# Attention, routed experts and a gated layer in one kernel: the first heads are split and loaded in another order, the row constants are cleared elsewhere, the first expert's row list is worked out inside the last attention steps, and one activation table set serves exponential and logarithm

## The reference

```python
def _attn_ref(q, k, v, tau):              # q, k, v: 4 x 8 heads x 576 x 64
    scores = scale * np.matmul(q, k.transpose(0, 1, 3, 2))
    thresh = np.max(scores, axis=-1, keepdims=True) - tau
    scores = np.where(scores >= thresh, scores, -1000000000.0)
    scores = scores - np.max(scores, axis=-1, keepdims=True)
    attn = np.exp(scores)
    attn = attn / (np.sum(attn, axis=-1, keepdims=True) + 1e-09)
    return np.matmul(attn, v)

def _moe_ref(x, w_gate, w_noise, noise, w1, w2):   # x: 2304 x 512, 8 experts of width 1024
    noise_scale = np.log1p(np.exp(x @ w_noise))
    noisy_logits = x @ w_gate + noise_scale * noise
    top2 = np.argpartition(-noisy_logits, 2, axis=1)[:, :2]
    ...
            h = np.maximum(x[mask] @ w1[e], 0.0)
            out[mask] += top2_w[mask, k, None] * (h @ w2[e])

def _moe2_ref(x, w_in, w_out, alpha):              # 2304 x 512, hidden width 2048
    h = x @ w_in
    g = np.maximum(h, 0.0) + alpha * np.minimum(h, 0.0)
    return g @ w_out
```

## Time and profile before

| what | value |
|---|---|
| runs, median | 1287.92 us (1285.68 to 1288.28, 3 runs) |
| the profiled execution's own time | 1287.75 us |
| its span, first to last instruction | 1285.5 us |
| busy: PE, PEld, DVE, ACT, POOL | 96%, 88%, 49%, 42%, 44% |
| first matmul of the kernel starts | 15.55 us after the span's start |
| last product of attention starts | 375.51 us |
| first expert matmul starts | 394.74 us |

### The profile page before, as it was taken

One profiled execution on the slowest core, in us unless ns is written; L12 is line 12 of the kernel. 1 busy time (PEld: TensorE's weight loads), 2 busy tenths in 40 slices (PEclk: granted clock), 3 DMA queues, 4 the chain that ended last, 5 costly groups with the idle time before them and its releaser, 6 DMA issues.

```text
span 1285.5 us, 20211 instructions
## 1 busy us (share of the span) xinstructions
PE 1232.2 (96%) x7666; PEld 1127.0 (88%) x7666; DVE 626.0 (49%) x1256; ACT 537.0 (42%) x957; POOL 569.6 (44%) x409
## 2 busy tenths in 40 slices
PE   4999999999988999999999999999999999999998
PEld 4899999999977789989999998998998999999997
DVE  6888888888777321121112121226455446445443
ACT  5777777777764333333333333323222112111211
POOL 5999999999651544352534434354510101000000
PEclk9999999999988999999999999999999999999999
DMA  5545454544421344342523434343221102000000
GB/s 172 133 123 138 124 142 122 139 123 122 139 68 58 102 144 132 99 138 92 164 76 119 122 123 132 113 153 121 90 67 49 33 1 74 16 0 24 17 1 24
DMA packets 71408, 123.11 MB, mean 96 GB/s; under 512 B 11936, under 2 KB 30880, under 8 KB 71328
## 3 DMA queue, kind: packets, MB, share of 16 engines
q1 hardware_dynamic: 57856, 87.69, 23.9%
q0 software_dynamic: 6080, 19.93, 4.9%
q10 hardware_dynamic: 7392, 14.42, 3.0%
HBM read 82.43 MB, written 19.92 MB: 80 GB/s over the span
## 4 chain that ended last, share of the span: by engine, by line
PE 79%; POOL 7%; ACT 4%; DMA 3%; DVE 3%; issue 3%; SPq 0%; ACTq 0%; DVEq 0%; POOLq 0%
PE h_ps L756 32%; PE y_ps L773 10%; PE y_ps L774 10%; PE y_ps L775 10%; PE o_acc L614 4%; POOL probs_lo L1429 4%; PE ring L565 2%; DMA qk_parts<-qk_parts 2%; PE t_ps L734 2%; PE ring L566 2%; PE ring L579 2%; PE ring L578 2%; POOL qk_parts L1434 1%; ACT probs_hi L867 1%; ACT qk_parts L875 1%
## 5 line engine op out<-in xcount | busy, mean ns | idle before, releaser
L756 PE MATMUL h_ps<-x_hi,region_a 128*128 128x384 f32 (+1 forms) x1408 | 340.0, 314 | 4.3 <-DVE x_lo L1325 4.3
L756 PEld LDWEIGHTS h_ps<-x_hi,region_a 128*128 128x128 f32 x1408 | 245.0, 189 | 10.1 <-DVE x_lo L1325 5.0
L1429 POOL TENSOR_TENSOR probs_lo<-probs,probs_hi 128x576 fp32r<-128x576 f32 x160 | 227.1, 1428 | 45.4 <-ACT probs_hi L867 45.2
L756 PE MATMUL h_ps<-x_lo,region_a 128*128 128x384 f32 (+1 forms) x704 | 219.3, 311 | 0.0
L1335 DVE SCALAR_TENSOR_TENSOR h_lo<-h_ps,h_hi 128x256 fp32r<-128x256 f32 (+1 forms) x128 | 62.7, 491 | 305.5 <-ACT h_hi L970 305.5
L973 ACT ACTIVATE h_hi<-act_out 128x384 fp32r<-128x384 f32 (+1 forms) x112 | 53.7, 480 | 305.9 <-DVE act_out L1346 305.9
L773 PE MATMUL y_ps<-region_b,h_hi 128*128 128x512 f32 x436 | 172.5, 396 | 1.4 <-DVE h_lo L1352 1.4
L775 PE MATMUL y_ps<-region_b,h_lo 128*128 128x512 f32 x436 | 170.8, 392 | 0.0
L774 PE MATMUL y_ps<-region_b,h_hi 128*128 128x512 f32 x436 | 170.7, 392 | 0.0
L1415 POOL TENSOR_TENSOR region_b<-stage,region_b 128x1024 fp32r<-128x1024 f32 x40 | 95.9, 2399 | 140.6 <-ACT region_b L848 140.5
L970 ACT ACTIVATE h_hi<-h_ps 128x256 fp32r<-128x256 f32 (+1 forms) x128 | 55.9, 437 | 237.7 <-PE h_ps L756 233.3
(11 more groups left out here) (247 smaller groups left out, 2404.4 us busy)
## 6 DMA issues: line engine op xcount, KB each, us to landing
stage<-in_moe_w SPq DMA_DIRECT2D x56, 512.0 KB, 3.7
qk_parts<-qk_parts SPq DMA_DIRECT2D x120, 160.0 KB, 2.5
qk_raw<-in_qk SPq DMA_DIRECT2D x32, 320.0 KB, 3.3
expert_rows<-rows_out ACTq DMA_DIRECT2D x8, 768.0 KB, 3.6
v_nat<-in_v SPq DMA_DIRECT2D x16, 320.0 KB, 3.2
early<-in_moe_w SPq DMA_DIRECT2D x16, 256.0 KB, 4.8
...
```

Source lines behind the costliest of these rows:

```text
L756: mm = pe.matmul(h_ps[:, c % 2, 0:width], wt, x[kind][:, cc, :], start=(n == 0), stop=(n == 3 * C - 1))
L1429: pool.tensor_tensor(probs_lo[:, m % 4, :], probs[:, m % 4, :], probs_hi[:, m % 4, :].bitcast(F32), ALU.subtract).then_inc(lo_done, 1)
```

## The change

1. **Filling.** Heads 0, 1 and 2 are split at slots -14, -13 and -11. The clearing of the constant rows of heads 2 and 3 goes from DVE to POOL, under a semaphore of its own (`later_row_consts`) for which PE waits only from head 2 on. The wait for `tau` goes from DVE's beginning to slot -4, and no longer counts in `consts_v`. ACT's last copy of a head moves one slot behind its split. SP loads the second pair of heads right after the first; the second pair's values and the fourth eighth of the weights come later. The weight eighths are split at other slots.
2. **Draining.** Pairs of row tiles are turned one slot earlier (`PAIR_AT` 144 in place of 145), while the first pairs are loaded in the same slot as before, 138. POOL writes its constants in slots 152 and 154. The counts (slot 162) go through a free place of `ring` and stand ahead of the turning of the last head. DVE works out the places in slots 161 to 163. Only two of the late turns stand ahead of the sum now, the rest behind it, and they wait for `first_idx_ready`.
3. **Table set.** ACT loads the set with exponential and logarithm once, at its beginning.

The diff, cut to its core:

```diff
-    PAIR_AT = TILES - 3 * NT
+    PAIR_AT = TILES - 16
...
-        SPLIT_AT = {-14: ((0, 0), (0, 1)), -9: ((1, 0), (1, 1)), -3: ((2, 0), (2, 1)), 2: ((3, 0),), 3: ((3, 1),)}
+        SPLIT_AT = {-10: ((0, 0), (0, 1)), -8: ((1, 0), (1, 1)), -1: ((2, 0),), 1: ((2, 1),), 3: ((3, 0),), 4: ((3, 1),)}
+        LOAD_FIRST_AT = {-5: 3}
+        FIRST_SPLITS = {-14: 0, -13: 1, -11: 2}
+        FIRST_COPIES = {-10: 2}
...
+        FIRST_COUNTS_AT = TILES - 1 + LAG
+        last_use = use("om", 0, NH + 1)
+        first_ps, marks_ps = (ring[:, (last_use + 1) % 3, a, :] for a in range(2))
...
             load_pair(0, 0)
+            load_pair(0, 2)
+            load_first_weights(0)
             sp.dma_start(threshold[:, :], tau.partition_broadcast(P)).then_inc(tau_in, 16)
-            load_first_weights(0)
             load_v_pair(0, 0)
-            load_pair(0, 2)
             load_first_weights(1)
             load_first_weights(2)
-            load_v_pair(0, 2)
-            load_first_weights(3)
...
-                for n, pairs in ((PAIR_AT - 7, range(0, 2)), (PAIR_AT - 1, range(2, PAIRS))):
+                for n, pairs in ((PAIR_AT - 6, range(0, 2)), (PAIR_AT - 1, range(2, PAIRS))):
...
             pe.wait_ge(consts, 2)
-            pe.wait_ge(consts_v, 3)
+            pe.wait_ge(consts_v, 2)
             pe.wait_ge(max_row_consts, 2)
...
                         wait(pe, copies_in[s % 2], copied(head(i, g)))
+                        pe.wait_ge(later_row_consts, 2)
...
+                if tile(i, c) == FIRST_COUNTS_AT:
+                    pe.wait_ge(freed, last_use - 1)
+                    pe.wait_ge(route_pool, 2)
+                    pe.wait_ge(first_mask_ready, 1)
+                    pe.matmul(first_ps[:, 0:FIRST_TILES], lower[:, :], first_mask[:, :], start=True, stop=False)
...
             pe.wait_ge(x_in[0], 16)
-            for k in range(4):
-                turn_late(k)
+            turn_late(0)
+            turn_late(1)
             pe.wait_ge(first_tokens_ready, 2)
...
             mm.then_inc(first_summed, 1)
+            pe.wait_ge(freed, past("om", 0, NH + 1))
+            pe.wait_ge(first_idx_ready, 1)
+            turn_late(2)
+            turn_late(3)
...
-                    if head(i, g) < BY_ENGINES:
-                        act.wait_ge(qk_hi_done, head(i, g) + 1)
-                        act.activation(k_ones[0:D, g % U, :], q_hi2[D:P, g % U, :].bitcast(F32), ACT.Copy).then_inc(highs_moved, 1)
-                        act.wait_ge(lows_moved, head(i, g) + 1)
-                        act.wait_ge(highs_moved, head(i, g) * 2 + 1)
-                        act.activation(k_parts[0:D, g % U, :], k_ones[0:D, g % U, :].bitcast(F32), ACT.Copy).then_inc(highs_moved, 1)
+                last = FIRST_SPLITS.get(tile(i, c) - 1)
+                if last is not None and last < BY_ENGINES:
+                    act.wait_ge(lows_moved, last + 1)
+                    act.wait_ge(highs_moved, last * 2 + 1)
+                    act.activation(k_parts[0:D, last, :], k_ones[0:D, last, :].bitcast(F32), ACT.Copy).then_inc(highs_moved, 1)
+                if g is not None and 0 <= head(i, g) < BY_ENGINES:
+                    act.wait_ge(qk_hi_done, head(i, g) + 1)
+                    act.activation(k_ones[0:D, g % U, :], q_hi2[D:P, g % U, :].bitcast(F32), ACT.Copy).then_inc(highs_moved, 1)
...
+            act.preload_act_table_set("natural_log_exp_and_others")
...
-            dve.wait_ge(tau_in, 16)
-
-            dve.tensor_scalar(threshold[:, :], threshold[:, :], -1.0 / SCALE, None, ALU.mult).then_inc(consts_v, 1)
...
+                if tile(i, c) == -4:
+                    dve.wait_ge(tau_in, 16)
+                    dve.tensor_scalar(threshold[:, :], threshold[:, :], -1.0 / SCALE, None, ALU.mult).then_inc(threshold_ready, 1)
...
                     if head(i, g) == BY_ENGINES - 1:
-                        max_rows_cleared(slice(2, U))
                         dve.wait_ge(max_row_consts, 2)
...
-                if tile(i, c) == FIRST_LOGITS_AT + 3:
+                if tile(i, c) == FIRST_COUNTS_AT - 1:
                     first_choice()
+                if tile(i, c) == FIRST_COUNTS_AT:
+                    first_expert_slots()
+                if tile(i, c) == FIRST_COUNTS_AT + 1:
+                    first_expert_places()
...
+            pool.memset(q_lo[D:D + 4, 2:U, :].bitcast(F32), 0.0).then_inc(later_row_consts, 1)
+            pool.memset(k_ones[D:D + 4, 2:U, :].bitcast(F32), 1.0).then_inc(later_row_consts, 1)
...
+                if tile(i, c) == PAIR_AT + 8:
+                    pool.wait_ge(pair_turned, 2)
+                    pool.memset(ones_bf[:, :], 1.0).then_inc(route_pool, 1)
```

180 lines of the change are left out of this document (94 added, 86 removed).

## The result

The changed kernel takes **1277.77 us** (median of 4 runs, 1276.27 to 1278.40) against 1287.80 us for the kernel before on the same chip (1285.68 to 1288.28): a ratio of 0.9924, with a 95% interval of 0.9906 to 0.9941. The profiled execution took 1278.40 us.

The account below looks back on a forecast made before the run. PE (95% busy) and POOL (91%) were taken to limit steady attention, so gains could come only from start and drain: 7.2 + 1.6 = 8.8 us off 1287.75, called 1279 us, range 1275.5 to 1283.5.

Parts of the forecast that it names:

- Start: First matmul: PE starts at 7.05 us, 8.5 us earlier, with 0.1 us allowed for a cast blocked by POOL's clearing.
- Rival (e): Start not won: slowed loads and blocking casts make PE start at 9.5 us; 1281.4 us in all, chance 0.09.
- Lead up to slot 0: Before attention's slot 0: row maxima reach ACT at 14.3 us; ACT finishes weight splits at 13.1, 1 us to spare.
- rival (a): Start won, but weight 1 lands at 15 us and ACT passes the wait on: 2.2 us lost, 1281.2 us, chance 0.12.
- Given back on POOL: POOL's unbroken stretch early in attention: one extra weight split, 1.26 us net, costs 1.3 us.
- Filling: Kernel's start as a whole: 8.5 us won less 1.3 us given back, 7.2 us saved.
- Table set: End of attention: without the load between exponential and logarithm, the last low part starts 0.94 us earlier.
- Drain: Last attention products to first expert matmul: 1.6 us saved, including the table load's 0.94; later steps keep their lengths.
- Rival (c): More than forecast: POOL's extra split finds slack (1.3 us), pairs return 1 us; 1276.7 us, chance 0.12.
- (b): Drain returns nothing: last heads' reload sets the end and the index wait holds PE's late turns; 1280.6 us, chance 0.10.
- From the span to the median: Whole kernel: a saving in the profiled span can be taken off the median as it is; 8.8 us off 1287.75.
- Slower by the clock (d): First score tiles: DVE stops PE, keeping its clock low; 1.4 us lost per tile, 1291.5 at nine; chance 0.04.

Follow-up runs that it names:

- the filling alone: Kernel before with only the start's edits (split, copy and load order, clearings on POOL, later threshold wait): 1279.54 us, ratio 0.9945.
- all but the filling: Kernel before with the table set, pairs a slot earlier and the new drain order, but the old start: 1284.48 us, ratio 0.9991.
- no table set: Changed kernel without the table set chosen at the start, so exponential and logarithm load their own sets: 1280.20 us, ratio 0.9949.
- pairs in their old slots: Changed kernel with the first pairs of rows turned one slot later, as in the kernel before: 1279.19 us, ratio 0.9939.
- the earlier split: Changed kernel with the third weight's second half split in slot -1, not 1: 1275.50 us; three more kernels add further edits: 1275.33, 1275.54, 1276.11 us.
- the second sitting: Changed kernel timed again, unaltered, beside the kernel before: 1279.10 against 1287.63 us, ratio 0.9931.

## Why the prediction was right, step by step

- **Start.** Forecast 7.05, measured 7.30. The forecast had PE start 3.32 us behind the landing of the first load, and it was 3.25; the load landed 0.32 us later. The 0.1 us for a blocked cast did not come: POOL's second clearing (1.16 us from 4.26, DVE's took 1.12) ended at 5.42, ahead of the cast at 5.68. Rival (e), 9.5, is out.
- **Lead up to slot 0.** Row maxima forecast at 14.3, measured 14.24. Weight 1 landed at 12.4, later than the estimate of 11 to 12, and ACT was through at 13.5, not 13.1. The spare 1 us was just enough; rival (a) was nearer than its 0.12 said.
- **Given back on POOL.** Forecast 1.26, and 1.25 by POOL's own rows. Filling: forecast 7.2; 7.30 at the low part of 38.72, and 7.0 for the filling alone at the last low part and the gather.
- **Table set.** Forecast 0.94; 0.93 at the last low part when it alone was added. That the first expert matmul moved by 0.94 as well was chance, as shown there. What the prediction missed is that the earlier soft terms would have put two loads on the path, and that the table set also pays for that.
- **Drain.** This is the step that failed in size: "From there the steps are as before". Turn 6 came at 378.39, forecast 378.3 on this clock. But from there to DVE's choice it took 3.12 us (381.51), and 2.26 before (385.80 to 388.06). PE did the late turns and logits at 1.2 GHz until about 380; turn 6 took 0.90 us, and 0.55 in the earlier trace rows. So the first expert matmul was at 386.80, not at 386.0, 7.9 us earlier and not 8.7. With all but the filling the clock was back up by 384.5, ahead of turn 6 at 385.40; from there to the choice it took 2.27 us, and every step came within 0.2 us of the forecast. Of the profiles with this order of the drain and the choice in its old place, three have PE at its upper clock at turn 6 (all but the filling, no table set, pairs in their old slots), and from turn 6 to the first expert matmul they take 7.56, 7.55 and 7.56 us; the four with PE at the lower level there take 7.92, 8.12, 8.40 and 8.41. So drain and table set together are worth what was forecast at an equal clock, and the clock took 0.86 us of it back in the changed kernel's profile.
- **Behind it.** The forecast had nothing here; the profile gained 0.8 us, 0.2 of it in the very first step and the rest because PE came back to 2.4 GHz 3.9 us after the first expert matmul, not 5.2. The sum of 8.8 was right because this and the failed step cancel, and that was luck. Rival (c) named this source ("if PE also kept its upper clock over the gap"). No rival named the loss: (b) expected one from the reload and the wait for the index, and both came when forecast.
- **From the span to the median.** The prediction took 8.8 us off the profiled execution's 1287.75. That execution's time fell by 9.35, 0.55 of it outside the span, and the median by 10.0. For these 1.2 us beyond the 8.8 the forecast has no term.
- **Slower by the clock (d).** This mechanism did not come: DVE did not stop PE, which ran without a gap from 7.30 to 13.2 us and came to its upper level at 11.5, 4.2 us after its start (before: 5.4, from 15.55 to 20.97). (The rival's own sum is off by one: 8.8 / 1.4 is 6.3, so it would have decided from seven tiles on.) Spells at a lower clock do come with the early start, but later, at 18 to 38 us, in 7 of 11 profiles. With the changed kernel's filling they cost 0.2 us at tile 60 on average, within the spread. With the earlier split tile 60 starts at 144.07 without a spell and at 144.67, 145.05 and 146.38 with one, so 0.6 to 2.3 us more, against a single profile without.

Still open: why the clock falls in the filling in some executions and not in others, with the same instructions. PE's busy time alone doesn't decide it: in the window from 18 to 22 us it was 2.61 us with a clock of 0.64 in one profile and 2.95 us at 1.00 in another. It is also open how much of the 10 us between the first medians is clock; 8.5 in the second sitting says that one or two of them may be.
